# Last batch of the mixer and router: y in the memory of val, codes scanned in PSUM, expert 0's second weights split by other engines, rows asked for without table reads

## The reference

```python
x = attention(q_pooled, k, v)                        # 4 x 8 heads, 576 x 1152 scores
h = relu(x @ w_in); u, v = halves(h)                 # mixer
v_s = w_spatial @ layer_norm(v) + b_spatial
y = (u * v_s) @ w_out
logits = y @ w_gate; local = sigmoid(y @ w_local)    # router
e[s] = argmax(logits[s]) if s == 0 or local[s] < 0.5 else e[s-1]
out[s] = softmax(logits[s])[e[s]] * (relu(y[s] @ w1[e[s]]) @ w2[e[s]])
```

## Time and profile before

| what | us |
|---|---|
| median of 3 runs | 1226.3 (1225.33 to 1229.69) |
| the profiled execution's own time | 1224.12 |
| its span | 1222.3 |
| PE busy | 1122.4 (92%) |
| DVE busy | 770.4 (63%) |
| ACT busy | 568.3 (46%) |
| POOL busy | 548.0 (45%) |

### The profile page before, as it was taken

One profiled execution on the slowest core, in us unless ns is written; L12 is line 12 of the kernel. 1 busy time (PEld: TensorE's weight loads), 2 busy tenths in 40 slices (PEclk: granted clock), 3 DMA queues, 4 the chain that ended last, 5 costly groups with the idle time before them and its releaser, 6 DMA issues.

```text
span 1222.3 us, 23724 instructions
## 1 busy us (share of the span) xinstructions
PE 1122.4 (92%) x7457; PEld 1031.1 (84%) x7458; DVE 770.4 (63%) x1457; ACT 568.3 (46%) x1044; POOL 548.0 (45%) x601
## 2 busy tenths in 40 slices
PE   6999999999999999999788999999608999799997
PEld 5999999999999999999678998989606788577785
DVE  3888888888888888888533272626344523452532
ACT  4666666666666666666242323324204411432411
POOL 6777777777777777775110010010243510440400
PEclk9999999999999999999879999999858999899998
DMA  5545443344544334443410103010326521541110
GB/s 185 143 144 154 147 136 107 93 141 144 154 145 140 104 94 141 144 115 96 138 39 1 39 19 129 0 39 1 108 83 219 185 86 34 196 133 44 34 38 27
DMA packets 68110, 125.94 MB, mean 103 GB/s; under 512 B 8238, under 2 KB 19630, under 8 KB 68080
## 3 DMA queue, kind: packets, MB, share of 16 engines
q1 hardware_dynamic: 38720, 53.01, 14.1%
q10 hardware_dynamic: 23376, 52.59, 13.8%
q0 software_dynamic: 5984, 19.95, 4.7%
HBM read 69.25 MB, written 57.33 MB: 104 GB/s over the span
## 4 chain that ended last, share of the span: by engine, by line
PE 38%; DVE 5%; issue 2%; DMA 2%; ACT 2%; POOL 1%; DVEq 0%; SPq 0%; POOLq 0%; ACTq 0%
PE second_ps L1585 10%; PE first_ps L1577 8%; PE wide L905 7%; PE tall L905 5%; PE tall L974 2%; PE small L974 2%; PE ht_ps L1569 1%; DMA rows_in<-sorted_tokens 1%; PE xt_ps L1562 1%; DMA sorted_tokens<-y,slot 1%; DVE w_l L1714 1%; DVE spatial_l L1254 1%; POOL sorted_tokens L868 1%; DVE val L1250 1%; ACT spatial_h L1122 1%
## 5 line engine op out<-in xcount | busy, mean ns | idle before, releaser
L639 DVE TENSOR_SCALAR_CACHE_REDUCE probs<-scores 128x1152 f32<-128x1152 f32 x144 | 195.4, 1357 | 62.4 <-PE scores L484 61.4
L484 PE MATMUL scores<-k_t,q_t 128*128 128x384 f32 x960 | 202.6, 348 | 1.3 <-DVE probs L639 1.3
L583 ACT ACTIVATE probs<-probs,neg_max 128x1152 f32<-128x1152 f32 x144 | 181.7, 1262 | 0.0
L614 ACT CAST pt_h<-ring 128x384 fp32r<-128x384 f32 x288 | 138.5, 481 | 74.0 <-PE ring L491 68.1
L507 PE MATMUL acc<-pt_h,v_parts 128*128 128x256 f32 (+1 forms) x576 | 169.1, 316 | 0.6 <-DVE pt_l L705 0.6
L491 PE MATMUL ring<-consts,probs 128*128 128x128 f32 x1296 | 165.4, 273 | 0.7 <-DVE pt_l L705 0.7
L484 PEld LDWEIGHTS scores<-k_t,q_t 128*128 128x128 f32 x960 | 161.5, 189 | 2.2 <-DVE probs L639 2.1
L507 PE MATMUL acc<-pt_l,v_parts 128*128 128x256 f32 (+1 forms) x576 | 157.2, 295 | 0.0
L340 POOL TENSOR_TENSOR pt_l<-mid,pt_h 128x384 fp32r<-128x384 f32 x144 | 145.4, 1010 | 12.0
L491 PEld LDWEIGHTS ring<-consts,probs 128*128 128x128 f32 x1296 | 146.4, 142 | 2.4 <-DVE pt_l L705 1.8
L705 DVE TENSOR_TENSOR pt_l<-ring,pt_h 128x384 fp32r<-128x384 f32 x288 | 145.6, 547 | 0.0
(11 more groups left out here) (212 smaller groups left out, 2551.0 us busy)
## 6 DMA issues: line engine op xcount, KB each, us to landing
sorted_tokens<-pad_row ACTq DMA_DIRECT2D x16, 2570.0 KB, 12.5
x_and_u<-moe_w POOLq DMA_DIRECT2D x10, 1024.0 KB, 6.1
k_nat<-k SPq DMA_DIRECT2D x32, 288.0 KB, 2.8
v_nat<-v SPq DMA_DIRECT2D x32, 288.0 KB, 4.7
q_nat<-q SPq DMA_DIRECT2D x32, 256.0 KB, 2.9
w_raw<-moe_w ACTq DMA_DIRECT2D x3, 2048.0 KB, 10.2
rows_in<-sorted_tokens SPq DMA_DIRECT2D x23, 257.0 KB, 2.7
x_heads<-x_pair SPq DMA_DIRECT2D x16, 256.0 KB, 4.1
```

The costliest lines, as they stand in the source:

```text
L484: mm = nc.tensor.matmul(scores[:, c, 0:CK], q_t[par][:, side, t * P:(t + 1) * P], k_t[par][:, c * CK:(c + 1) * CK], start=(i == 0), stop=( ...
L583: nc.scalar.activation(probs[n % 3][:], probs[n % 3][:], ACT.Exp, bias=neg_max[:, n % 3:n % 3 + 1], scale=-1.0, accum_out=row_sum[:, n:n + ...
L614: nc.scalar.copy(pt_h[:, 3 * c:3 * c + 3, n * P:(n + 1) * P], ring[c][:, 0:CK].rearrange("p (i r) -> p i r", i=3)).then_inc(s["high_done"], 1)
L639: nc.vector.tensor_scalar(probs[n % 3][:], scores[:, :, 0:CK], -0.5 * DH ** -0.5, None, ALU.mult, ALU.min, accum_out=neg_max[:, n % 3:n % ...
```

## The change

Six edits:

1. In the last batch, y is written into the memory of `val` (now `val_space`, made wide enough) instead of that of `y`, and ACT no longer waits for `y_free` but for two older events of val's users.
2. In all batches, the two `small` banks become one tile of two halves; `spread` writes the codes there as 2 x 288 columns (tile t = 2 straddles the halves, so six products instead of five), and the scan reads them in PSUM: the two copies go, the chain's scan is done in two halves.
3. The scan's rows of the last batch lie in `gated` and `bsp` instead of in `val`.
4. ACT's four casts of expert 0's w2 move from behind the last batch's copies of y to between them: pieces 0 and 1 behind tile 1, piece 2 behind tile 2, piece 3 behind tile 3. Each waits for its piece to land.
5. The low parts of expert 0's w2 are made by DVE, between those of w1 and `choose` of the last batch, instead of by POOL.
6. SP waits for the last scatter behind its reads of the table, at each load of rows, instead of ahead of them. POOL's first load of the next expert's w2 waits for the first rows to be loaded instead of for the scatter.

```diff
@@ -749,7 +749,8 @@
     x_h, x_l = (shared["x_parts"][:, i * KD * TP:(i + 1) * KD * TP].rearrange("p (k s) -> p k s", k=KD)
                 for i in range(2))
     wout_raw = u_t[:, :, 0:DM]
-    val = sb("val", [P, QT, FH])
+    val_space = sb("val", [P, QT * YW])
+    val = val_space[:, 0:QT * FH].rearrange("p (t n) -> p t n", t=QT)
     val_h, val_l = (shared["spatial_" + part][:, QT * T:].rearrange("p (t n) -> p t n", t=QT) for part in "hl")
     stats = sb("stats", [P, QT, 6])
     moments = sb("moments", [P, QT, 2])
...
@@ -759,9 +760,9 @@
     gated = [sb(f"gated{i}", [P, T]) for i in range(2)]
     gate_h = sb("gate_h", [P, KD, TP], F32R)
     gate_l = sb("gate_l", [P, KD, TP], F32R)
-    y = sb("y", [P, QT, YW])
-    logits = y[:, :, DM:DM + E + 1]
-    wout_t = y[:].rearrange("p t c -> p (t c)")[:, 0:KD * DM].rearrange("p (k n) -> p k n", k=KD)
+    y_space = sb("y", [P, QT, YW])
+    y_last = val_space[:].rearrange("p (t c) -> p t c", t=QT)
+    wout_t = y_space[:].rearrange("p t c -> p (t c)")[:, 0:KD * DM].rearrange("p (k n) -> p k n", k=KD)
     top = sb("top", [P, QT])
     under = sb("under", [P, QT, E])
     key = sb("key", [P, QT, E])
...
@@ -776,8 +777,14 @@
     prob = sb("prob", [P, QT, E])
     chosen = sb("chosen", [P, QT, E])
 
-    scan_rows = val[0:E].rearrange("p t n -> p (t n)")
-    codes, keeps, chain, ranks = (scan_rows[:, i * T:(i + 1) * T] for i in range(4))
+    def y_of(b):
+        return y_last if isinstance(b, int) and b == B - 1 else y_space
+
+    def scan_rows(b):
+        if isinstance(b, int) and b == B - 1:
+            return gated[0][0:E], gated[1][0:E], bsp[0:E]
+        return tuple(val_space[0:E, i * T:(i + 1) * T] for i in range(3))
+
     onehot = sb("onehot", [E, T])
     carry = sb("carry", [E, 1])
     place = sb("place", [E, TP])
...
@@ -788,7 +795,9 @@
     ahead = sb("ahead", [E, 2])
     at_place = sb("at_place", [E, LIST])
 
-    small = [pb(f"small{i}", [P, 512]) for i in range(2)]
+    smalls = pb("smalls", [P, 2, 512])
+    small = [smalls[:, i] for i in range(2)]
+    codes = smalls[0:E, :, 0:HT]
     wide = [pb(f"wide{i}", [P, 2, 512]) for i in range(2)]
     tall = [pb(f"tall{i}", [P, 512]) for i in range(2)]
 
...
@@ -868,17 +877,12 @@
                 pool.indirect_dma_start(
                     out=sorted_dram,
                     out_offset=bass.IndirectOffsetOnAxis(ap=slot[0:rows, t:t + 1], axis=0),
-                    in_=y[0:rows, t, 0:ROW], in_offset=None).then_inc(s["scattered"], 16)
+                    in_=y_of(b)[0:rows, t, 0:ROW], in_offset=None).then_inc(s["scattered"], 16)
 
         with pool.Fori(0, B - 1) as b:
             scatter(b)
             pool.wait_ge(s["scattered"], 16 * QT * (b + 1))
             pool.sem_inc(s["y_free"], 1)
-        for piece in range(PIECES):
-            part = slice(2 * piece, 2 * piece + 2)
-            pool.wait_ge(s["w2_hi"], piece + 1)
-            nc.gpsimd.tensor_tensor(w2_l[:, part], w2_raw[:, part], w2_h[:, part].bitcast(F32), ALU.subtract
-                                    ).then_inc(s["w2_lo"], 1)
         scatter(B - 1)
 
 
...
@@ -1017,9 +1021,11 @@
 
             pe.wait_ge(s["code_ready"], b + 1)
             for t in range(QT):
-                rows = rows_of(t)
-                out = small[1][0:E, t * P:t * P + rows] if t < QT - 1 else small[0][0:E, 0:rows]
-                mm = nc.tensor.matmul(out, code8[:, t], ident[:, 0:rows], start=True, stop=True)
+                for half in range(2):
+                    a, e = max(t * P, half * HT), min(t * P + rows_of(t), (half + 1) * HT)
+                    if a < e:
+                        mm = nc.tensor.matmul(codes[:, half, a - half * HT:e - half * HT], code8[:, t],
+                                              ident[:, a - t * P:e - t * P], start=True, stop=True)
             mm.then_inc(s["spread_done"], 1)
 
         def placed(b):
...
@@ -1133,13 +1139,18 @@
                 act.wait_ge(s["gated_ready"], KD * b + m + 1)
                 nc.scalar.copy(gate_h[:, m, 0:T], gated[m % 2][:]).then_inc(s["gate_hi"], 1)
 
-        def project(b):
+        def project(b, last=False):
             for t in range(QT):
                 act.wait_ge(s["y_done"], QT * b + t + 1)
-                if t == 0:
+                if t == 0 and last:
+                    act.wait_ge(s["val_lo"], B)
+                    act.wait_ge(s["scan_step"], RANK * b + 1)
+                elif t == 0:
                     act.wait_ge(s["y_free"], b + 1)
-                nc.scalar.copy(y[:, t, 0:YA], tall[t % 2][:, 0:YA])
-                nc.scalar.copy(y[:, t, YA:YW], small[t % 2][:, 0:YA]).then_inc(s["y_ready"], 1)
+                nc.scalar.copy(y_of(b)[:, t, 0:YA], tall[t % 2][:, 0:YA])
+                nc.scalar.copy(y_of(b)[:, t, YA:YW], small[t % 2][:, 0:YA]).then_inc(s["y_ready"], 1)
+                if last and 1 <= t < QT - 1:
+                    first_high(((), (4, 5), (6,), (7,))[t])
 
         def soften(b):
             act.wait_ge(s["under_ready"], b + 1)
...
@@ -1198,9 +1209,8 @@
         with act.Fori(0, B - 2) as b:
             batch(b, True)
         batch(B - 2, False)
-        project(B - 1)
+        project(B - 1, True)
         soften(B - 1)
-        first_high(range(PIECES, 2 * PIECES))
 
     def vector_program(dve):
         nc.vector.memset(x_in[REM:P, QT - 1], 0.0).then_inc(s["zeroed"], 1)
...
@@ -1312,10 +1323,15 @@
 
             dve.wait_ge(s["val_lo"], splits)
             dve.wait_ge(s["spread_done"], b + 1)
-            nc.vector.tensor_copy(codes[:, 0:MAIN], small[1][0:E, 0:MAIN])
-            then(nc.vector.tensor_copy(codes[:, MAIN:T], small[0][0:E, 0:REM]))
-            then(nc.vector.tensor_scalar(keeps, codes, 0.0, None, ALU.is_equal))
-            then(nc.vector.tensor_tensor_scan(chain, keeps, codes, 0.0, ALU.mult, ALU.add))
+            keeps, chain, ranks = scan_rows(b)
+
+            def halved(row):
+                return row.rearrange("p (h c) -> p h c", h=2)
+
+            then(nc.vector.tensor_scalar(halved(keeps), codes, 0.0, None, ALU.is_equal))
+            then(nc.vector.tensor_tensor_scan(chain[:, 0:HT], keeps[:, 0:HT], codes[:, 0], 0.0, ALU.mult, ALU.add))
+            then(nc.vector.tensor_tensor_scan(chain[:, HT:T], keeps[:, HT:T], codes[:, 1], chain[:, HT - 1:HT],
+                                              ALU.mult, ALU.add))
             then(nc.vector.tensor_scalar(onehot[:], chain, const("expert1", E), None, ALU.is_equal))
             then(nc.vector.tensor_tensor_scan(ranks, onehot[:], onehot[:], carry[:], ALU.add, ALU.max))
             then(nc.vector.scalar_tensor_tensor(
...
@@ -1381,6 +1397,11 @@
             dve.wait_ge(s["w1_hi"], piece + 1)
             nc.vector.tensor_tensor(w1_l[:, piece], w1_raw[:, piece], w1_h[:, piece].bitcast(F32), ALU.subtract
                                     ).then_inc(s["w1_lo"], 1)
+        for piece in range(PIECES):
+            part = slice(2 * piece, 2 * piece + 2)
+            dve.wait_ge(s["w2_hi"], piece + 1)
+            nc.vector.tensor_tensor(w2_l[:, part], w2_raw[:, part], w2_h[:, part].bitcast(F32), ALU.subtract
+                                    ).then_inc(s["w2_lo"], 1)
         choose(B - 1)
         rank(B - 1, B)
 
...
@@ -1473,6 +1494,7 @@
         def load_rows(g, row):
             sp.wait_ge(s["tag_taken"], g + 1)
             sp.wait_ge(s["x_turned"], g + 1)
+            sp.wait_ge(s["scattered"], 16 * QT * B)
             sp.dma_start(rows_in[:], sorted_dram[bass.ds(row, P)]).then_inc(s["rows_loaded"], 16)
 
         def place(j, par):
...
@@ -1483,7 +1505,6 @@
                     load_rows(before + i, expert * CAP + i * P + 1)
 
         sp.wait_ge(s["counts_ready"], 1)
-        sp.wait_ge(s["scattered"], 16 * QT * B)
         places(sp, place)
 
         total = entry(sp, TILES, 0)
...
@@ -1514,7 +1535,7 @@
             pool.dma_start(w2_raw[:, part], w2_d[expert][:, part]).then_inc(half_loaded[half], 16)
 
         pool.wait_ge(s["counts_ready"], 1)
-        pool.wait_ge(s["scattered"], 16 * QT * B)
+        pool.wait_ge(s["rows_loaded"], 16)
         with pool.If(entry(pool, IN_USE, 1) > 0):
             for half in range(2):
                 load2(1, entry(pool, EXPERT, 1), half)
```

More of the change, by code:

```diff
@@ L1277, in then @@
                 dve.wait_ge(s["route_step"], n[0])
+            logits = y_of(b)[:, :, DM:DM + E + 1]
             l8 = logits[:, :, 0:E]
@@ L1334, in tag @@
             nc.vector.tensor_copy(slot[:], out[:, :, E]).then_inc(s["y_tagged"], 1)
-            nc.vector.tensor_copy(y[:, :, DM + 1].bitcast(I32), tokens[:]).then_inc(s["y_tagged"], 1)
+            nc.vector.tensor_copy(y_of(b)[:, :, DM + 1].bitcast(I32), tokens[:]).then_inc(s["y_tagged"], 1)
             dve.wait_ge(s["counted"], 2 * b + 1 + 1)
-            nc.vector.tensor_reduce(y[:, :, DM], chosen[:], AX.X, ALU.add).then_inc(s["y_tagged"], 1)
+            nc.vector.tensor_reduce(y_of(b)[:, :, DM], chosen[:], AX.X, ALU.add).then_inc(s["y_tagged"], 1)
```

## The result

Before: 1227.99 us, the median of 4 runs (1225.33 to 1230.15). Changed: 1215.99 us, the median of 4 (1211.82 to 1216.32). The ratio is 0.9895, with an interval of 0.9863 to 0.9928: 12.0 us faster, where 17.9 were forecast. Timed again later on another chip, the changed kernel took 1212.32 (6 runs, 1210.44 to 1216.26) beside 1225.79 for the kernel before (11 runs, 1224.90 to 1232.56): 0.9886, with an interval of 0.9863 to 0.9909, 13.5 us faster. The profiled execution took 1216.16.

The account below looks back on a forecast made before the run. It took a serial chain of waits at the end of routing, with PE idle from 863.5 us, as the bound. 8.0 + 3.3 + 3.6 - 0.4 + 3.4 + 3.0 - 3.0 = 17.9 off 1226.3 gave 1208.4 us, range 1204 to 1213.5.

Parts of the forecast that it names:

- step 5: Loads after the first rows: w1 of expert 1 leaves together with w2, takes 11.0 us, PE waits; 3.0 us lost.
- rival B: Collision is dear: w1 lands 14 us after issue, PE falls to the low clock, 2.3 more; 1213.7 us; chance 20%.
- Step 3: Last batch's scan to the one-hot: comparison from PSUM 0.75, two half-scans 0.75 each; 3.6 us gained.
- Step 4: After the last scatter: table read earlier, 3.4 us gained; first rows travel alone, 2.7 instead of 5.67, 3.0 gained.
- Step 1: Last batch's y copies no longer wait for a scatter; `choose` starts at 874.0 instead of 882.03, 8.0 us gained.
- Step 2: `choose` to the scan, last batch, without POOL beside it: 3.15 instead of 6.46; 3.3 us gained.
- sixth product of `spread`: In PE's stream in batches 0 to 2, at most 0.23 us, three times; 0.4 us lost (0.1 to 0.7).
- 11.0 beside 1 MB: Argument against the dear collision: a w1 load issued beside a 1 MB load of POOL's and one of rows took 11.0.
- 11.7: w1 of expert 1 if queues take turns, half of 391 GB/s while w2 lasts: loss 3.7, 1209.1 us in all.

Follow-up runs that it names:

- e5: Changed kernel with the last batch's y back in y's memory and ACT's old wait for `y_free`; 1222.43 us.
- e4: Changed kernel with the second half of expert 1's w2 asked for only when its w1 has landed; 1207.48 us.
- c2: Changed kernel run again unaltered, for times on another chip and a second trace; median 1212.32 us, ratio to before 0.9886.
- e1: Changed kernel with POOL asking for expert 1's w2 when the last scatter has landed, not the first rows; 1210.94 us.
- e3: Changed kernel with ACT asking for expert 1's w1 at the last scatter's landing, ahead of the cast of the first rows; 1204.50 us.
- e3t: e3 again, timed with 5 runs; median 1207.15 us, ratio to before 0.9833.
- e8: e3 plus 36 unread transposes filling PE's gap near 667 us, against the changed kernel; median 1207.11 us, ratio to before 0.9833.
- e6: Changed kernel with the four low parts of expert 0's w2 back on POOL, the casts staying between the copies; 1217.45 us.

## Why the prediction was off

The sign was right, and so was the mechanism of the collision; the size failed at **step 5, "I take 11.0"** for w1 of expert 1, with no low clock behind the wait: 3.0 lost were forecast and 8.9 measured, since w1 took 14.3 and PE's clock fell. What happened is rival B. Steps 3 and 4 have the right numbers, in part for wrong reasons. Term by term, each measured between events of the same region, so that a clock drawn earlier drops out:

| step | forecast gain | trace of before to changed |
|---|---|---|
| 1. y in val's memory | 8.0 | 8.6 (`choose` to `choose` 55.50 to 46.91); e5 undoes it: 8.9 |
| 2. `choose` to the scan | 3.3 | 2.9 (6.46 to 3.55) |
| 3. scan | 3.6 | 3.6 (5.96 to 2.39) |
| 3. sixth product of `spread` | -0.4 | 0.0 (batches 63.5 and 63.6 apart in both traces) |
| 4. table reads | 3.4 | 3.4 (one-hot to the rows' issue 17.95 to 14.54) |
| 4. the rows' landing | 3.0 | 2.9 |
| 5. collision | -3.0 | -8.9 (rows landed to first result 18.28 to 27.15) |
| not forecast | | 1.7 (first to second result 14.02 to 12.36), -1.1 in what follows |
| sum | 17.9 | 13.1 |

13.1 stands well to the measured 12.0 and 13.5. In the pair of spans only 7.9 is seen, because the changed kernel's execution lost 5.2 to its clock ahead of the region and that of before nearly nothing (82.57 is the shortest of all the traces).

**Step 5 in detail.** Its mechanism (both loads leave together, three casts and the second turned half hang on w1, PE's gap follows) is in the trace as told. The size came from a load with 1 MB beside it, and here there are 2. e4, with 1 MB, gave 11.4, close to the row's 11.0; with 2 MB it took 14.1 to 15.2 in five traces. The low clock, which the forecast had at 0 and rival B at 2.3, came too: PE waited 6.5 in one piece, and 12 matmuls took 5.42 instead of 2.84, 2.6 more (1.8 more in c2, behind 6.66). That term was missing by itself: in e4, with w1 near the forecast's 11.0, PE's wait of 3.34 was still followed by the low clock (0.66 granted from 917.3 to 921.7), and from the rows' landing to the first result it took 23.2, which is 4.9 lost and not 3.0. B put w1 at 14 us and the total at 1213.7; the ten timed runs of the changed kernel in both sets have their middle at 1213.1. The argument against B, "11.0 beside 1 MB", spoke for it: the megabyte more had to be added. By turns between the queues (the Trainium skill, "DMA: Bandwidth & Descriptors", section "Queues, rings and completion order") I had worked out 11.7. The growth with POOL's bytes, 8.9, 11.4, 14.3, agrees with turns taken, as it would with any even sharing. The 11.7 started from a w1 that has its own queue to itself; in the trace ACT issues the 2 MB for expert 2 at 907.82, while w1 is still under way, and without any of POOL's bytes w1 already takes 8.9. Add to 8.9 the 2 MB at 391 GB/s, 5.4 us, and 14.3 comes out; this sum was made afterwards, and from the 7.8 of the kernel before, which has the same load 2.8 us behind w1, it would give 13.2. How the two loads of ACT's queue share it was not tried apart, nor why it was 15.2 once, so that part of the size stays open.

**Step 1** was right for a slightly wrong reason: I had `choose` wait for the last low part of w2; it waits for y, 0.32 later. **Step 2** lost 0.4 at `spread`, 1.05 of waiting for which DVE shows in its row. That was the clock: `spread` took 1.62 at a granted 0.67 there, and 1.16 at 1.00 in c2, where 3.08 passed from `choose` to the scan, as forecast; so the sixth product costs next to nothing (five took 1.15). **Step 3** has the right sum and the wrong giver: it set the 3.6 down to the new form of the scan, and batch 2 shows 0.3 for that and 3.3 for POOL's absence, which it had counted in step 2 only. Its single terms came out: the comparison from PSUM took 0.75, as worked out, where SBUF gave 0.45, as the Trainium skill ("VectorE: DVE Perf Modes", section "Why PSUM operands drop a tier") has it; the half-scans took 0.74 and 0.80. (The 3.8 that the step names, if the comparison keeps 0.45, should read 3.9, as further on in it.) **Step 4** took POOL's later loads for the reason why the rows land in 2.7; e1, without that half of edit 6, has them in 2.64. The 1.7 that was not forecast is DVE's pair of `w_l` operations after the first result: 2.36 in the changed kernel, 4.54 in that of before, where POOL was making low parts (5.81 from 936.10) at the same time. It comes with the lateness: in e3, where w1 is in time, the pair takes 4.54 again and the second result comes 14.11 after the first. I had not looked past the first result.

**The clock.** The forecast set one trace of before against its median and had no term for what such a trace draws. All traces together: 82.6 to 88.3 us from batch 0's norm to its `choose`, so a single pair can err by 5.7, nearly half of what was to be measured. What makes the clock fall behind the same gap in one execution and not in another stays open.

## What to carry to other kernels

When an edit makes two large loads leave together, price the one that is waited for by the bytes that share its time, and add the megabytes to the nearest row instead of taking that row as it is. Look for loads behind it in its own queue too, though their share was not measured here. The cure is then an order, not a size: here, asking 4.3 us sooner for the load that is needed first took back 5 us, and asking 7.5 us sooner still ran into the scatters. Ask also what holding a load back gains: here it gained nothing. When one edit takes an engine away from beside another, read the undisturbed time from a stretch where that engine is idle, before a gain is credited to a second edit. Compare two traces by distances between events inside the region of the change, and profile each kernel twice before a difference of a few microseconds is explained.

## What was not expected of the hardware

- A load of 2 MB took 7.8 to 8.9, 11.4 and 14.1 to 15.2 us with 0, 1 and 2 MB of another engine's queue beside it; issued 3.5 us ahead of those 2 MB it took 8.3, 8.7 and 9.3 (e3, e3t, e8).
- A gap of PE of 2.87 us at the same place is followed by the 2.4 GHz level in some executions of a program and by the 1.2 GHz level in others.
- While POOL subtracts, DVE operations of 5 and 40 elements took 2.00 and 2.22 us (e6) and neighbours of the same size 0.20: a stretched one ends with POOL's operation beside it, and some pass. What lets one pass was not tried apart.
